# Two slots instead of four for token and gate, earlier weight splits and a merged tail in the expert loop

## What is computed

```
logits = x @ w_gate                        # x: 1536 tokens x 384
expert_idx = argmax(logits, axis=1)
gate_w = softmax(logits)[token, expert_idx]
# the first `capacity` = 384 tokens of each expert go to disp[e, pos]
h = maximum(einsum('ecd,edf->ecf', disp, w1), 0.0)      # 384 -> 1024
y = einsum('ecf,efd->ecd', h, w2)                       # 1024 -> 384
out[i] = gate_w[i] * y[expert_idx[i], pos[i]]           # 0 where not kept
```

## Time and profile before

| | us |
|---|---|
| median of 3 runs | 426.72 (426.27 to 426.89) |
| the profiled execution | 426.89 |
| its span | 425.2 |
| TensorE busy, matmuls | 404.5 (95%) |
| VectorE busy | 259.1 (61%) |
| ScalarE busy | 192.7 (45%) |
| GpSimd busy | 230.5 (54%) |
| the expert stage, from expert 0's remainder to the end | 289.6 to 425.2 |

### The profile page before, as it was taken

How to read it: one execution, slowest core, us unless ns; L and a number is a source line. 1 busy time by engine, 2 the same in 40 slices (tenths; PEclk the granted TensorE clock), 3 DMA queues, 4 the chain that set the end, 5 groups by cost and what they waited for, 6 DMA issues and landing times.

```text
span 425.2 us, 9305 instructions
## 1 busy us (share of the span) xinstructions
PE 404.5 (95%) x3194; PEld 388.3 (91%) x3195; DVE 259.1 (61%) x523; ACT 192.7 (45%) x442; POOL 230.5 (54%) x239
## 2 busy tenths in 40 slices
PE   5799999999999999999999999999998999999893
PEld 5688899999999999999999999998988999899782
DVE  6888877665426334364343888563967484834960
ACT  2889955431311113111132243335858576536851
POOL 3999817563323633236353596054949375518862
PEclk9999999999999999999999999999999999999997
DMA  6997027428960100001000256039977575817501
GB/s 241 404 382 224 3 76 217 138 93 272 371 242 2 37 19 0 0 0 37 19 0 0 79 178 187 22 98 337 313 247 214 181 236 181 273 40 215 192 9 31
DMA packets 34331, 61.76 MB, mean 145 GB/s; under 512 B 4798, under 2 KB 27310, under 8 KB 34288
## 3 DMA queue, kind: packets, MB, share of 16 engines
q1 hardware_dynamic: 31280, 55.92, 40.1%
q0 software_dynamic: 3008, 5.29, 3.6%
HBM read 47.92 MB, written 15.18 MB: 148 GB/s over the span
## 4 chain that ended last, share of the span: by engine, by line
PE 72%; DVE 10%; issue 5%; PEld 4%; ACT 4%; POOL 3%; DVEq 0%; DMA 0%; ACTq 0%; POOLq 0%; PEldq 0%
PE bank L1418 24%; PE bank L1379 23%; PE bank L1632 4%; DVE w_low L1166 3%; PE bank L1363 3%; PE bank L1327 2%; PE bank L1355 2%; PE bank L1601 2%; ACT w_high L801 2%; PE bank L1702 2%; PE bank L1519 2%; PEld bank L1632 2%; DVE expert_g_low L1159 1%; PE bank L1652 1%; PE bank L1313 1%
## 5 line engine op out<-in xcount | busy, mean ns | idle before, releaser
L554 POOL TENSOR_TENSOR g_low<-act_full,g_high 128x384 fp32r<-128x384 f32 x63 | 65.2, 1034 | 111.2 <-ACT g_high L708 111.2
L708 ACT ACTIVATE g_high<-act_full 128x384 fp32r<-128x384 f32 x64 | 33.7, 526 | 146.6 <-DVE act_full L1041 134.0
L1379 PE MATMUL bank<-x_split,w_high 128*128 (+1 forms) x384 | 98.6, 338 | 0.2 <-DVE w_low L954 0.2
L1035 DVE TENSOR_SCALAR neg<-bank,alpha_sb 128x384 f32<-128x384 f32 x64 | 39.4, 616 | 89.2 <-PE bank L1379 89.2
L636 POOL TENSOR_TENSOR w_low<-w_raw,w_high 128x384 fp32r<-128x384 f32 x48 | 52.7, 1134 | 34.8 <-ACT w_high L801 34.8
L1379 PEld LDWEIGHTS bank<-x_split,w_high 128*128 128x128 f32 x384 | 68.9, 188 | 0.9 <-DVE w_low L954 0.5
L1418 PE MATMUL bank<-w_high,g_high 128*128 128x384 f32 x189 | 64.5, 341 | 0.0
L1379 PE MATMUL bank<-x_split,w_low 128*128 (+1 forms) x192 | 64.5, 336 | 0.0
L1418 PE MATMUL bank<-w_low,g_high 128*128 128x384 f32 x189 | 63.9, 338 | 0.0
L1418 PE MATMUL bank<-w_high,g_low 128*128 128x384 f32 x189 | 63.9, 338 | 0.0
L1041 DVE SCALAR_TENSOR_TENSOR act_full<-bank,neg 128x384 f32<-128x384 f32 x64 | 35.7, 557 | 2.4
(11 more groups left out here) (171 smaller groups left out, 852.3 us busy)
## 6 DMA issues: line engine op xcount, KB each, us to landing
w_raw<-chunks SPq DMA_DIRECT2D x96, 192.0 KB, 4.4
w_raw<-chunks SPq DMA_DIRECT2D x32, 384.0 KB, 3.7
rk_in<-att_rk SPq DMA_DIRECT2D x12, 704.0 KB, 6.1
routed_rows<-fill SPq DMA_DIRECT2D x1, 5211.0 KB, 18.1
xe<-routed_rows SPq DMA_DIRECT2D x7, 579.0 KB, 4.4
v_in<-att_v SPq DMA_DIRECT2D x12, 200.0 KB, 5.8
out<-fill SPq DMA_DIRECT2D x1, 2304.0 KB, 23.3
x_split<-x_split POOLq DMA_DIRECT2D x18, 48.0 KB, 2.7
```

Of the source, the lines that this page charges most:

```text
L554: pool.tensor_tensor(gl[:, f % 4, :], act_full[:, f % 2, :], gh[:, f % 4, :].bitcast(f32), ALU.subtract).then_inc(s_gl, 1)
L708: act.activation(gh[:, f % 4, :], act_full[:, f % 2, :], ACT.Copy).then_inc(s_gh, 1)
L1035: dve.tensor_scalar(neg[:, f % 2, :], h, 0.0, alpha_sb[:, f:f + 1], ALU.min, ALU.mult)\
L1379: last = mm(bank[f % 4][:, 0:G], a[:, f, w], x[:, kc, bass.ds(g * G, G)], start=kc == 0 and i == 0, stop=kc == KC - 1 and i == 2)
```

## The change

Four edits, all in the expert stage.

1. `token` and `gate` have two slots instead of four, indexed by `e % 2`. `keep_meta(e)` waits for `s_gone` of max(e - 1, 0) + 1 instead of max(e - 3, 0) + 1.
2. On ScalarE, in expert 0, `split_high(31)` moves ahead of the first `flip_high`. On VectorE `split_low` of chunks 29 to 31 moves between the two `flip_relu` of expert 0.
3. On TensorE, in a one-tile expert, `s_w1free` and `no_tile(1)` follow the second turn instead of preceding it, and `s_fh[2]` and `no_tile(2)` are raised ahead of the second layer.
4. On TensorE the second layer of the last tile of a one-tile and of a two-tile expert becomes one shared block behind the first branch. Both use `flip_down(e, 0, b)`; before, a two-tile expert used `expert_down(e, 0, b)`.

```
-            for c in range(2 * NF - 3, 2 * NF - 1):
+            for c in range(2 * NF - 3, 2 * NF):
                 split_high(c)
             flip_high(0, 0, (0,))
             xe_high(1, 0, bank[X_BANK[0]])
-            split_high(2 * NF - 1)
             flip_high(0, 0, (1,))
...
-                dve.wait_ge(s_gone, max(e - 3, 0) + C_GONE)
-                dve.tensor_copy(token[:, e % 4, :], xe[:, e % 2, :, DM:DM + 1].rearrange("p a b -> p (a b)"))
+                dve.wait_ge(s_gone, max(e - 1, 0) + C_GONE)
+                dve.tensor_copy(token[:, e % 2, :], xe[:, e % 2, :, DM:DM + 1].rearrange("p a b -> p (a b)"))
...
             flip_relu(0, 0, 0)
+            for c in range(2 * NF - 3, 2 * NF):
+                split_low(c)
             flip_relu(0, 0, 1)
             flip_low(0, 0, 0)
             xe_low(1, 0, bank[X_BANK[0]])
             flip_low(0, 0, 1)
             for i in range(1, GT):
                 xe_low(1, i, bank[X_BANK[i]])
-            for c in range(2 * NF - 3, 2 * NF):
-                split_low(c)
             keep_meta(1)
...
                             turn_xe(e + 1, i, bank[X_BANK[i]], 1 - b)
-                    pe.sem_inc(s_w1free, 1)
+                    flip_turn(e, 0, (1,))
                     no_tile(1)
-                    flip_turn(e, 0, (1,))
-                    flip_down_high(e, 0, 0, b)
-                    pe.sem_inc(s_fh[2], 2)
-                    no_tile(2)
-                    flip_down_low(e, 0, 0, b)
-                    flip_down_high(e, 0, 1, b)
-                    flip_down_low(e, 0, 1, b)
-                    pe.sem_inc(s_ft[2], 2)
                 with pe.Else():
...
                     expert_down(e, 1, b)
-                    with pe.If(rows < 2 * P + 1):
-                        pe.sem_inc(s_w1free, 1)
-                        pe.sem_inc(s_fh[2], 2)
-                        no_tile(2)
-                        expert_down(e, 0, b)
-                        pe.sem_inc(s_ft[2], 2)
-                    with pe.Else():
...
+                with pe.If(rows < 2 * P + 1):
+                    pe.sem_inc(s_w1free, 1)
+                    pe.sem_inc(s_fh[2], 2)
+                    no_tile(2)
+                    flip_down(e, 0, b)
+                    pe.sem_inc(s_ft[2], 2)
+                with pe.Else():
...
```

24 lines of the change are left out of this document (12 added, 12 removed).

## The result

| | before | changed |
|---|---|---|
| median | 426.81 us | 431.6 us |
| runs | 426.27 to 426.98 | 429.95 to 433.21 |
| ratio to before, 95% interval | | 1.0105 [1.0072, 1.0139] |
| profiled execution | 426.89 us | 429.56 us |
| its span and mean granted clock | 425.2 us, 0.995 | 427.9 us, 0.996 |

The account below looks back on a forecast made before the run. TensorE was taken to bound the kernel. Ring 8.4 + splits 1.1 + tail 0.5 + clock 1.0 = 11.0 us on 426.7 gave 437.7 us, 2.6% slower; range for 8 in 10: 433.3 to 443.

Parts of the forecast that it names:

- TensorE bounds the kernel, and its waits add up: Whole kernel: TensorE is busy 404.5 of 425.2 us, so any time it waits is added nearly one for one.
- GpSimd raises that only inside its turn for the same expert e, after its eight subtracts for w1 of expert e+2.: Flag that VectorE's `keep_meta(e+1)` awaits with two slots: dated by GpSimd's first scatter, so VectorE stands 8.4 us at `keep_meta(3)`.
- G: Start of GpSimd's first scatter of the turn, 0.16 us after its last subtract, taken as the flag's time; D + 6.8.
- D: Start of TensorE's first block in a two-tile expert; the fifth block would have started at D + 4.56.
- fourth rival: Not slower: flag up before TensorE needs VectorE, subtracts ended before D + 3.9, ring costs nothing; 425.0 us, chance 0.03.
- The sign of being right: VectorE's cast of `keep_meta(e+1)` starts with GpSimd's first scatter of expert e, some 8 us of idle ahead.
- The ring, 8.4: Two slots for token and gate: 1.1, 3.6, 0.4 and 3.3 us over experts 1 to 6; from 6.7 to 11.3.
- The moved splits, 1.1: Expert 0: TensorE waits 1.4 us before its second turn, 0.30 given back; net 1.1, from 0.3 to 1.6.
- The merged tail, 0.5: TensorE, one-tile experts: a new taken jump in three experts, 0.5 us for all; bounds 0 and 3 x 2.03.
- the sign of being wrong: Among others, TensorE idle without a releaser between the second turn and `flip_down` in experts 5 to 7.
- The rival with 2 us or more for each stall: Jump stalls: expert 7 and perhaps the loop's pair wait for code, 439.5 to 442 us; chance 0.11.
- The clock, 1.0: Expert 6: almost 5 us of TensorE idle brings the lower clock for a short while; 1.0, between 0 and 6 us.

Follow-up runs that it names:

- flag_after_subtracts: The changed kernel with one more GpSimd wait, for the completion count of its eight subtracts, ahead of the flag `s_gone`; 445.94 us, 1.0422 of before.
- after_third: The changed kernel run once more, unaltered; 431.53 us, 1.0117 of before.
- merge_look: The kernel before with edits 3 and 4 alone (TensorE's merged tail), run once more for its trace; 429.72 us.
- four_slots_again: The changed kernel with four slots for token and gate and the early flag (edits 2, 3 and 4), run a second time; 429.68 us, 1.0057 of before.
- merge_only: The kernel before with edits 3 and 4 alone, TensorE's merged tail; 429.64 us, 1.0047 of before.
- splits_behind_lows: The kernel before with one chunk's split instead of two between VectorE's two `flip_relu` in one-tile experts, other splits behind `xe_low`; 428.94 us, 1.0044 of before.
- unmerged: The kernel before with the changed kernel's order of last-tile products and increments, but each branch keeping its own copy; 428.44 us, 1.0019 of before.

## Why the prediction was wrong, step by step

- **TensorE bounds the kernel, and its waits add up.** Right for the bound: TensorE's last product ends 2.66 us later, and the profiled execution took 2.67 more. The bracketed waits grew by only 0.6, so waits had to be read from the starts.
- **"GpSimd raises that only inside its turn for the same expert e, after its eight subtracts for w1 of expert e+2."** This is the step that failed. The order in the program is right. That order was taken for order of completion, and G was dated by the first scatter, which does wait for the engine. The flag comes 0.16 us behind ScalarE's last `split_high1`, at D + 2.56 in expert 3 (D = 338.33) and not at D + 6.8. The waits it led to are real once the premise is: with a flag that waits for the subtracts, `flag_after_subtracts` has VectorE's 7.64, TensorE's 2.68 to 3.08 before the fifth blocks and the 5.36 in expert 6, where 2 to 3 and "almost 5" were forecast. Their prices were not sound: that kernel is 18.1 us slower than before and not 11.0, with three falls of the clock where one was priced. (A small part is that the "about 5.0" from the fifth block to the second layer is 5.2 by its own rows.) The prediction's fourth rival named the right condition, a G before D + 3.9, and was refused because "nothing in the edit starts the subtracts earlier"; it was their end that did not matter. The sign of being right that it had named, the cast starting with GpSimd's first scatter, did not come: the cast starts 4.4 us before it.
- **The ring, 8.4.** Measured: 1.0 alone, and on top of the other edits 1.9 in one comparison, 1.3 to 1.6 by the traces. Per two-tile expert it is 0.49 and not 1.8, alone in two experts, since expert 2 starts late there anyway, and in three with the merge. That anything is lost with the flag at D + 2.56 is a second step that failed: cast and copy were put at 0.2, by which `relu_low` would have ended at D + 3.2, ahead of the fifth block. They took 1.96 from the flag to `relu_low` (340.89 to 342.85), in the midst of GpSimd's subtracts; `relu_low` then ends 0.4 late. In expert 6 nothing of the 3.3 came.
- **The moved splits, 1.1.** Right: 1.2 measured. The wait at the second turn, forecast as 1.4, was between 0.52 and 2.31 in the ten traces with this edit (0.83, 1.47, 1.55 and 1.85 among them). So the term scatters by more than its size between executions, with the landing of the last chunks: ScalarE's last `split_high` but one waits for its load until 291.95 in the first trace, 294.11 in `after_third` and 294.64 where the 2.31 stand. That is the larger part of what the changed kernel's other traces have over its first: the turn came at 296.25 there and at 297.47 in `after_third`, which ended 1.8 us later (422.26 against 420.50).
- **The merged tail, 0.5.** Too small: 2.3 measured. Between the second turn and `flip_down` 2.0 us are added, 1.2 with the branch, in expert 7 as in the loop, and 0.8 with the order, which was priced at nothing; 0.9 us come back at expert 2. The rest of the 2.3 lies in executions that left no trace. The waits ahead of `flip_down` are the sign of being wrong that the prediction had named for these experts. It had compared the branches to one behind a dozen products (338.24 without a gap), while here four transposes of 0.66 us stand ahead, which it had noted and not priced. The rival with 2 us or more for each stall was wrong as well. By the Trainium skill's rule on fetches (Runtime: NRT & Kernel Launch, section Instruction fetch mechanics) the loop's pair would pay nothing and expert 7 a fetch. The traces have 0.19 and 0.62 in the loop and 0.53 in expert 7, and their DMA records show no wait for a fetch: of the instruction queue q8, 16 KB a packet, the changed kernel has no packet from 337.4 to 416.1, all through experts 3 to 6, and the next starts at 416.10, with the first product of `flip_down` in expert 7, and takes 0.99 us while the products run on. (That q8 is TensorE's is inferred: only TensorE's code has the loop over which it is silent.)
- **The clock, 1.0.** This was for the wait of 5 us that didn't come. In the changed kernel's four traces, all at 0.995 or above, no fall shows before the end. But two of the four executions of its median are at 0.992 and 0.993 and took 433 us. They left no trace; `merge_look` and `four_slots_again`, at 0.993, have a fall in expert 6, and by `merge_only`'s two groups it is worth 1.3 us of an execution that meets it, less than the 3 us that lie between the two pairs here. So the clock probably has a share in the merge's price that the prediction had put beside the ring; what else the executions at 433 met is open.

Sum: 1.0 for the ring alone, up to 1.9 on top, + 1.2 + 2.3 = 4.5 to 5.4, against 3.1, 4.2 and 4.8 measured. The forecast of 11.0 was right in sign and in the term of the splits: 6.5 to 7.4 too much for the ring and 1.0 for the clock stand against 1.8 too little for the tail.

## What to carry to other kernels

A semaphore that a sequencer raises by itself behind compute instructions, as GpSimd's does here, says that they have been handed on, not that they have ended: date it by the last wait ahead of it in that queue, here ScalarE's last split, and hang it on the compute instruction if completion is meant. Before a branch is put between a short piece of work and a long one, look at how much is queued ahead of it on that engine: behind 0.66 us of transposes one cost 0.35 to 0.5 us here, behind a dozen products nothing was seen. And where a profiled execution is the quickest of its kernel, its waits explain less than the median has.

## What was not expected of the hardware

- GpSimd's flag preceded the end of the work ahead of it by 4.3 us (340.89 against 345.16), while it never preceded the moment at which the last subtract's own input was ready: 0.15 or 0.16 us after it in five of five places.
- A cast and a copy of 128x3 elements took 0.17 and 0.16 us behind GpSimd's subtracts, and 1.06 and 1.07 in the midst of them. Right at their start it was 0.79 and 0.16 (337.15 and 337.85 before), so not every operation pays. Subtracts of 128x384 on GpSimd took 7.83 us for eight with VectorE waiting, 8.18 to 8.87 beside VectorE's, 9.48 in expert 5.
- The granted clock fell behind waits of 3.08 and 2.70 us, at the end of one of 2.31, within one of 5.36, and behind 1.47 + 0.62, and stayed at full behind 2.68, behind 2.70 in `splits_behind_lows`, and behind another 1.47 + 0.62 in `merge_only`. Each of the nine falls ahead of the last product took 1.7 us of clock. What decides between equal waits is open. `unmerged` and `splits_behind_lows` had a fall in 10 to 14 us, far from all edits, where before had none.
- Why the 2.03 us ahead of expert 2 go in kernels with the shorter loop body, and stay in those without (1.02 to 1.72 ahead of the product there, 1.71 before), was seen in all traces but not tried apart.
